# A fused spectral mixer and feed-forward kernel: three edits of the order of work (turning of a tile, mixing tables and first rows, third weight chunk)

## The chip, the core and the metric

The kernel runs on one core of one Trainium2 chip. The metric is the device time of the core in microseconds (us), as the median of several runs. The engines are TensorE (PE in the rows, PEld its weight loads), VectorE (DVE), ScalarE (ACT), GpSimd (POOL) and SyncE (SP), which here only issues DMAs. Each engine works through its own list in order, and they meet at semaphores.

## The reference

Two stages, both in float32:

```python
X = rfft(x, axis=1)                     # x: 4 x 3008 x 256
Yr = Xr @ w_r - Xi @ w_i + b_r          # complex mixing over the 256 features
Yi = Xr @ w_i + Xi @ w_r + b_i
Y  = soft_threshold(Yr, 0.01) + 1j * soft_threshold(Yi, 0.01)
y  = irfft(Y, n=3008, axis=1)           # 12032 rows of 256
h  = y @ w_in                           # 256 -> 2048
g  = max(h, 0) + alpha * min(h, 0)
out = g @ w_out                         # 2048 -> 256
```

## The kernel before, in words

Every product is made of three matmuls in a rounded format: a value is split into an upper part (`_hi`, mostly a ScalarE copy) and the rest (`_lo`, a subtraction on VectorE or GpSimd), and hi*hi, hi*lo and lo*hi are summed in PSUM.

The feed-forward stage is a loop over 24 tiles `f` (6 for each of the 4 batches, 502 or 500 rows of y each) and, in a tile, over 16 steps `m` of 128 hidden units. On TensorE a step is `hidden(f, m)` (6 matmuls into one of two banks `h_ps`) and, two steps behind (`LAG = 2`), `output` (3 matmuls into each of the two halves of `out_ps`). Between them lie, for step m: ScalarE's `bend` (`rows<-h_ps`, the negative part), VectorE's `bend` (`g_raw`), ScalarE's `split_bent` (`g_hi`), VectorE's `rest_bent` (`g_lo`). When the 16 steps are summed, VectorE turns the two halves of `out_ps` (`turn(f-1, 0)` and `turn(f-1, 1)`, `turned<-out_ps`) at step 1 of the next tile, and `output(f, 0)` may overwrite the first half after turn 0 and the second after turn 1.

The Fourier transforms of the next batch are woven into these steps. The order is written out by hand in each engine's loop, with functions that say what lies at which step: `s_unit` (first forward stage: `x_hi`, `x_lo`, `forward1`, `copy_fwd` into `staging`), `p_unit` and `p_couple` (second stage, mixing), `i_unit` (inverse: `inverse1`, `split_y`, `rest_y`), `i_bpair` (pairs of rows to be loaded by `load_back` and split). The split of a pair of rows is `split_back` on ScalarE (lines 850, 851), `rest_back` on GpSimd (line 1288, of `inv_sb`) and `rest_first` on VectorE (line 1129, of the 32 first rows). Batch 0's transform is done ahead of the loop, in the head.

`ffw` is the pair of weights `w_in`, `w_out`, cut in 8 chunks of 2 steps. SyncE loads a chunk into one of two places in `turned` (`load_ffw`, lines 431 and 433); ScalarE makes `win_hi` and `wout_hi`, VectorE `win_lo` (`rest_win`), GpSimd `wout_lo` (`rest_wout`). In tile 0, chunk `m // 2 + 2` is split at each even step m. `load_ffw(w)` waits until chunks 0 to w - 2 have their rests. The sums and differences of the mixing weights for the later batches are made on GpSimd at tile 1, step 0, and split by `split_mixw` (ScalarE) and `rest_mixw` (GpSimd). Rests on VectorE have line 991, those on GpSimd line 1239.

Of the kernel before, what the change touches and what calls it, by code (L numbers as in the profile page):

```python
# [62 lines left out]
LAG = 2  # L63
PERIOD = 6 * STEPS
CHUNKS = 8

ALONE = (1, TILES * STEPS - 1)


# [36 lines left out]

def i_split(f, m):

    return i_bpair(f, 0) if m == 2 else i_bpair(f, m - 1) if m > 2 else None


def i_bpair(f, m):

    pairs = next_bpairs(f)
    return pairs[m // 4] if m % 4 == 0 and m // 4 < len(pairs) else None


def mixer_kernel(nc, x, w_r, w_i, b_r, b_i, w_in, w_out, alpha, dft, idft, twiddles, out):
    with ExitStack() as ctx:
# [227 lines left out]
        def _(sp):  # L347
# [125 lines left out]

            for f in range(TILES):
                for m in range(STEPS):
                    if f == 0 and m % 2 == 0 and m >= 2:
                        load_ffw(m // 2 + 3)
                    if f == 0 and m == STEPS - 1:
                        sp.wait_ge(win_lo_done, CHUNKS)
                        sp.wait_ge(wout_lo_done, CHUNKS)  # L480
                        sp.wait_ge(itw_lo_done, GROUPS)
                        for c in range(2):
                            sp.dma_start(ffw_raw(1)[:, c * 2 * DIM:(c + 1) * 2 * DIM].rearrange("p (h e) -> p h e", h=DH),
                                         (w_r, w_i)[c].rearrange("(h p) e -> p h e", h=DH)).then_inc(mixw_again, 16)
                            sp.dma_start(bias_both[:, c, :], (b_r, b_i)[c].rearrange("(o e) -> o e", o=1).to_broadcast([P, DIM])
                                         ).then_inc(both_loaded, 16)
                    if f >= 1 and 4 <= m < 10:
                        store_out(sp, f - 1, 2 * (m - 4))
                        store_out(sp, f - 1, 2 * (m - 4) + 1)
                    s = s_unit(f, m)  # L490
                    if s is not None:
                        store_fwd(sp, s)
                        load_x(s + X_RING)
                    if f % 6 == 1 and m == 2 and f < TILES - 6:
                        for j in range(4):
                            load_pair(PAIRS * (f // 6 + 1) + j)
                    p = p_unit(f, m, 0)
                    if p is not None:
                        if p % PAIRS + 4 < PAIRS:
                            load_pair(p + 4)  # L500
                    p = p_unit(f, m, 2)
                    if p is not None and p % 3 == 0:
                        load_table(p // 3 + 1)
                    p = p_couple(f, m, 6)
                    if p is not None:
                        store_couple(p)
                    v = i_bpair(f, m)
                    if v is not None:
                        load_back(v)
# [235 lines left out]
        def _(act):  # L745
# [185 lines left out]
                split_back(v)  # L931
            for u in HEAD_ORDER:
                split_y(u)
            act.wait_ge(win_hi_done, 2)
            act.wait_ge(wout_hi_done, 2)
            for f in range(TILES):
                for m in range(STEPS):
                    q = f * STEPS + m
# [8 lines left out]
                    s = s_unit(f, m)  # L947
                    if s is not None:
                        copy_fwd(s)
                    if f == 1 and m in (1, 2):  # L950
                        split_mixw(m)
                    p = p_couple(f, m, 5)
                    if p is not None:
                        copy_couple(p)
# [12 lines left out]
                    v = i_split(f, m)  # L967
                    if v is not None:
                        split_back(v)
                    if f == 0 and m % 2 == 0 and m // 2 + 2 < CHUNKS:  # L970
                        split_ffw(m // 2 + 2)
                    p = p_unit(f, m, 0)
                    if p is not None:
                        split_whole(p)
# [14 lines left out]
        def _(dve):  # L989
# [191 lines left out]
                    split_x(S_HEAD + (k - 19) // 2, True)  # L1181
            for s in range(S_HEAD + 2, S_EARLY):
                split_x(s, True)
            for v in range(HEAD_V):
                rest_back(v)
            for u in HEAD_ORDER:
# [5 lines left out]
            for f in range(TILES):  # L1192
                for m in range(STEPS):
                    if f >= 1 and m == LAG - 1:
                        turn(f - 1, 0)
                    q = f * STEPS + m
                    if q in ALONE:
                        rest_bent(*divmod(q - 1, STEPS))
                    bend(f, m)
                    p = p_unit(f, m, 0)  # L1200
                    if p is not None:
                        whole_spec(p)
                    if q >= 1 and q not in ALONE:
                        rest_bent(*divmod(q - 1, STEPS))
                    if f >= 1 and m == LAG - 1:
                        turn(f - 1, 1)
# [14 lines left out]
                    p = p_unit(f, m, 0)  # L1221
                    if p is not None:
                        rest_whole(p)
                    if f == 0 and m % 2 == 0 and m // 2 + 2 < CHUNKS:
                        rest_win(m // 2 + 2)
                    p = p_couple(f, m, 3)
                    if p is not None:
                        rest_couple(p)
                    v = i_bpair(f, m - 2)
                    if v is not None:  # L1230
                        rest_first(v)
            rest_bent(TILES - 1, STEPS - 1)
# [4 lines left out]
        def _(pool):  # L1237
# [70 lines left out]
            for p in (PAIRS - 2, PAIRS - 1):  # L1308
                for b in (4, 5):
                    hand_over(pool, p, b, head_handed)  # L1310
            pool.wait_ge(wout_lo_done, 2)
            for f in range(TILES):
                for m in range(STEPS):
                    p = p_unit(f, m, 0)
# [2 lines left out]
                    if f == 1 and m == 0:  # L1317
                        make_mixw(1)
                        make_mixw(2)
                    if f == 1 and m in (1, 2):  # L1320
                        rest_mixw(m)
                    p = p_unit(f, m, -2)
                    if p is not None and p % 3 == 0:
                        rest_tw(p // 3)
# [6 lines left out]
                    p = p_unit(f, m, 0)  # L1331
                    if p is not None:
                        rest_sum(p)
                    if f == 0 and m % 2 == 0 and m // 2 + 2 < CHUNKS:
                        rest_wout(m // 2 + 2)
                    if s_unit(f, m + 2) is not None:
                        rest_x(s_unit(f, m + 2))
            for n in (9, 10, 11):
# [68 lines left out]
```

## Time and profile before

| | us |
|---|---|
| median of 3 runs | 1391.45 (1390.62 to 1391.94) |
| the profiled execution | 1391.81 |
| its span, first to last instruction | 1389.8 |
| TensorE busy in it | 1365.3 |
| VectorE, ScalarE, GpSimd busy | 1028.2, 763.1, 318.5 |
| mean granted TensorE clock | 0.994 |

The profiled execution is one run; its own time is 0.36 us over the median, and 2.0 us of it lie outside the span. Durations in this text come from that execution.

### The profile page before, as it was taken

The page shows a single profiled execution, that of the slowest core. Times are in us where ns is not written, and L with a number is a line of the kernel's source. Part 1 is how long each engine was busy: PE and PEld are TensorE (multiplying, and loading weights), DVE is VectorE, ACT ScalarE, POOL GpSimd, SP SyncE. Part 2 cuts the span into 40 slices and gives each one's busy share as a digit, 9 for nine tenths or more (in the row PEclk, how much of TensorE's full clock was granted, in tenths as well). Part 3 has the DMA queues.
Part 4 walks back from the last instruction along what each step waited for, and adds up shares of the span by engine and source line. Part 5 has one row for each costly group of instructions (what it writes and reads, how often), then busy time and mean ns, then how long its engine had stood idle before and what let it go on. Part 6 is the DMA issues. An engine that isn't in the chain of part 4 may idle for free.

```text
span 1389.8 us, 21671 instructions
## 1 busy us (share of the span) xinstructions
PE 1365.3 (98%) x6906; PEld 1156.2 (83%) x6906; DVE 1028.2 (74%) x1887; ACT 763.1 (55%) x1709; POOL 318.5 (23%) x361
## 2 busy tenths in 40 slices
PE   7999999999999999999999999999999999999997
PEld 4987888888888888888888888888888888888886
DVE  6776788888866768989876667888886566566654
ACT  4775566665644555666644545666564444444443
POOL 1443432332200422333210332323220000000000
PEclk9999999999999999999999999999999999999999
DMA  8654532232211542323211343232311121102101
GB/s 257 180 152 138 156 86 72 74 80 84 53 44 31 145 126 60 81 71 83 59 49 42 82 116 86 66 79 77 87 43 41 28 49 39 24 26 49 27 16 15
DMA packets 174700, 106.85 MB, mean 77 GB/s; under 512 B 112198, under 2 KB 150390, under 8 KB 174587
## 3 DMA queue, kind: packets, MB, share of 16 engines
q1 hardware_dynamic: 170755, 101.64, 27.4%
q10 hardware_dynamic: 3608, 3.66, 0.8%
q8 instruction: 56, 0.92, 0.3%
q14 instruction: 57, 0.47, 0.1%
q0 software_dynamic: 224, 0.16, 0.1%
HBM read 67.87 MB, written 37.49 MB: 76 GB/s over the span
## 4 chain that ended last, share of the span: by engine, by line
PE 92%; DVE 4%; issue 1%; ACT 1%; DMA 1%; POOL 0%; SPq 0%; POOLq 0%; DVEq 0%; ACTq 0%
PE out_ps L525 39%; PE h_ps L525 37%; PE work_ps L525 11%; PE work_ps L631 2%; PE work_ps L559 1%; PE work_ps L633 1%; DVE x_lo L991 1%; DVE g_lo L991 1%; PE work_ps L560 1%; DVE g_raw L1092 1%; DVE turned L1146 0%; DVE x_hi L999 0%; PE h_ps L690 0%; DMA room<-in_twiddles_dram 0%; DVE shr_lo L991 0%
## 5 line engine op out<-in xcount | busy, mean ns | idle before, releaser
L865 ACT ACTIVATE rows<-h_ps 128x502 f32<-128x502 f32 (+1 forms) x384 | 225.8, 588 | 522.0 <-PE h_ps L525 522.0
L1092 DVE SCALAR_TENSOR_TENSOR g_raw<-rows,keep,h_ps 128x502 f32<-128x502 f32 (+1 forms) x384 | 280.9, 732 | 271.5 <-ACT rows L865 267.6
L525 PE MATMUL out_ps<-g_hi,wout_hi 128*128 128x502 f32 (+1 forms) x768 | 307.3, 400 | 3.0 <-DVE g_lo L991 2.0
L525 PE MATMUL h_ps<-y_hi,win_hi 128*128 128x502 f32 (+1 forms) x768 | 300.7, 392 | 0.1
L525 PE MATMUL h_ps<-y_lo,win_hi 128*128 128x502 f32 (+1 forms) x768 | 300.3, 391 | 0.0
L525 PE MATMUL out_ps<-g_hi,wout_lo 128*128 128x502 f32 (+1 forms) x768 | 299.8, 390 | 0.0
L525 PE MATMUL h_ps<-y_hi,win_lo 128*128 128x502 f32 (+1 forms) x768 | 299.3, 390 | 0.0
L525 PE MATMUL out_ps<-g_lo,wout_hi 128*128 128x502 f32 (+1 forms) x768 | 299.0, 389 | 0.0
L991 DVE TENSOR_TENSOR g_lo<-g_raw,g_hi 128x502 fp32r<-128x502 f32 (+1 forms) x384 | 273.6, 713 | 1.0 <-ACT g_hi L874 0.7
L874 ACT ACTIVATE g_hi<-g_raw 128x502 fp32r<-128x502 f32 (+1 forms) x384 | 236.9, 617 | 1.7 <-DVE g_raw L1092 1.7
L525 PEld LDWEIGHTS out_ps<-g_hi,wout_hi 128*128 128x128 f32 x768 | 144.9, 189 | 33.6 <-DVE g_lo L991 10.0
L525 PEld LDWEIGHTS h_ps<-y_hi,win_hi 128*128 128x128 f32 x768 | 145.5, 189 | 30.9 <-issue 0.5
L525 PEld LDWEIGHTS h_ps<-y_hi,win_lo 128*128 128x128 f32 x768 | 144.8, 189 | 30.9
L525 PEld LDWEIGHTS out_ps<-g_hi,wout_lo 128*128 128x128 f32 x768 | 144.8, 189 | 30.1
L525 PEld LDWEIGHTS h_ps<-y_lo,win_hi 128*128 128x128 f32 x768 | 145.1, 189 | 29.7
L525 PEld LDWEIGHTS out_ps<-g_lo,wout_hi 128*128 128x128 f32 x768 | 145.6, 190 | 21.1
L1239 POOL TENSOR_TENSOR back_lo<-inv_sb,back_lo 128x256 fp32r<-128x256 f32 x61 | 54.5, 893 | 414.3 <-ACT back_lo L851 414.3
L1261 POOL TENSOR_TENSOR room<-room 128x128 f32<-128x128 f32 x72 | 60.1, 835 | 324.8 <-DVE room L1015 324.8
L1239 POOL TENSOR_TENSOR x_lo<-x_raw,x_hi 94x512 fp32r<-94x512 f32 x44 | 59.2, 1346 | 89.6 <-DVE x_hi L999 89.6
L525 PE MATMUL work_ps<-mixw_hi,spec_hi 128*128 128x256 f32 x216 | 61.5, 285 | 0.0
L525 PE MATMUL work_ps<-mixw_lo,spec_hi 128*128 128x256 f32 x216 | 61.0, 282 | 0.0
L525 PE MATMUL work_ps<-mixw_hi,spec_lo 128*128 128x256 f32 x216 | 60.9, 282 | 0.0
(143 smaller groups left out, 2007.8 us busy)
## 6 DMA issues: line engine op xcount, KB each, us to landing
pair_raw<-fwd_scratch SPq DMA_DIRECT2D x96, 128.0 KB, 2.2
rows<-inv_scratch SPq DMA_DIRECT2D x61, 192.0 KB, 2.4
table<-in_twiddles_dram SPq DMA_DIRECT2D x28, 384.0 KB, 3.4
inv_scratch<-inv_sb SPq DMA_DIRECT2D x36, 256.0 KB, 2.2
x_raw<-in_x_dram SPq DMA_DIRECT2D x56, 160.0 KB
fwd_scratch<-staging SPq DMA_DIRECT2D x46, 192.0 KB, 2.1
inv_sb<-inv_scratch SPq DMA_DIRECT2D x122, 64.0 KB, 2.3
out_dram<-turned SPq DMA_DIRECT2D x124, 40.0 KB, 1.8
```

Of the source, the lines that this page charges most:

```text
L525: mm = pe.matmul(ps, lhs, rhs, start=(first and n == 0), stop=(last and n == len(terms) - 1), **kw)
L559: pe.matmul(both, hi, tw.rearrange("p w c -> p (w c)"), start=True, stop=False, skip_group_check=True)
L560: mm = pe.matmul(both[:, 0:P], lo, tw[:, 0, :], start=False, stop=True, skip_group_check=True)
L631: pe.matmul(i_bank(u)[:, b * 2 * NA:(b + 1) * 2 * NA], back_hi[:, v % 2, d], parts, start=b == 0, stop=False, skip_group_check=True)
L633: pe.matmul(i_views(u)[0], back_lo[:, v % 2, h * P:(h + 1) * P], idft_rest[:, :, :], start=False, stop=True, skip_group_check=True).then_i ...
L865: act.activation(negpart[:, q % 2, 0:size], h_ps[:, q % 2, 0:size], ACT.Relu, scale=-1.0).then_inc(negpart_done, 1)
L874: act.activation(g_hi[:, q % 3, 0:size], g_raw[:, q % 2, 0:size], ACT.Copy).then_inc(g_hi_done, 1)
L991: return dve.tensor_tensor(dst, whole, hi.bitcast(F32), ALU.subtract)
L1092: dve.scalar_tensor_tensor(g_raw[:, q % 2, 0:size], negpart[:, q % 2, 0:size], keep[:, m:m + 1], h_ps[:, q % 2, 0:size], ALU.mult, ALU.add ...
L1239: return pool.tensor_tensor(dst, whole, hi.bitcast(F32), ALU.subtract)
L1261: pool.tensor_tensor(spec_sum, spec[:, :, 0, :], spec[:, :, 1, :], ALU.add).then_inc(sum_done, 1)
```

## The change

Four things are moved; no arithmetic is added or dropped.

1. At step 1 of each tile from 1 on (`m == LAG - 1`), VectorE makes `g_lo` of the step before ahead of `g_raw` of this one.
2. The mixing tables are split at steps 3 and 4 of tile 1, not 1 and 2. The first pair of rows of tile 0 is split at step 3, not 2.
3. The third weight chunk (number 2) is split by VectorE alone in the head, ahead of `rest_back`, and not at step 0 of tile 0.
4. In tile 0, step m issues the load of chunk m/2 + 4 from step 0 on, where before it was chunk m/2 + 3 from step 2 on.

```diff
+FFW_HEAD = 3
 def i_split(f, m):
-    return i_bpair(f, 0) if m == 2 else i_bpair(f, m - 1) if m > 2 else None
+    first = 3 if f == 0 else 2
+    return i_bpair(f, 0) if m == first else i_bpair(f, m - 1) if m > first else None
+def i_first(f, m):
+    return i_bpair(f, 0) if m == (3 if f == 0 else 2) else i_bpair(f, m - 2) if m > 2 else None
+def ffw_unit(f, m):
+    w = m // 2 + 2
+    return w if f == 0 and m % 2 == 0 and FFW_HEAD <= w < CHUNKS else None
...
 # sync
-                    if f == 0 and m % 2 == 0 and m >= 2:
-                        load_ffw(m // 2 + 3)
+                    if f == 0 and m % 2 == 0:
+                        load_ffw(m // 2 + 4)
...
 # scalar
-            act.wait_ge(win_hi_done, 2)
-            act.wait_ge(wout_hi_done, 2)
+            act.wait_ge(win_hi_done, FFW_HEAD)
+            act.wait_ge(wout_hi_done, FFW_HEAD)
...
-                    if f == 1 and m in (1, 2):
-                        split_mixw(m)
+                    if f == 1 and m in (3, 4):
+                        split_mixw(m - 2)
...
-                    if f == 0 and m % 2 == 0 and m // 2 + 2 < CHUNKS:
-                        split_ffw(m // 2 + 2)
+                    w = ffw_unit(f, m)
+                    if w is not None:
+                        split_ffw(w)
...
 # vector
+            for step in range(4):
+                split_ffw(2, step)
             for v in range(HEAD_V):
                 rest_back(v)
...
-                    if q in ALONE:
+                    g_first = q in ALONE or m == LAG - 1
+                    if g_first:
                         rest_bent(*divmod(q - 1, STEPS))
                     bend(f, m)
...
-                    if q >= 1 and q not in ALONE:
+                    if q >= 1 and not g_first:
                         rest_bent(*divmod(q - 1, STEPS))
...
-                    v = i_bpair(f, m - 2)
+                    v = i_first(f, m)
                     if v is not None:
                         rest_first(v)
```

GpSimd's `rest_wout` and `rest_mixw` and VectorE's `rest_win` follow in the same way.

Three places show how the lists of the engines differ; the changed kernel's lines lie 14 to 19 further down. The first is SyncE's queue in tile 0, steps 0 to 4, in the kernel before. A line with `turned` is half of a weight chunk's load, the group of `rows` and `inv_sb` is one `load_back`.

```order
L406 DMA rows<-inv_scratch 96x512 [waits inv_stored_1,inv_stored_2,inv_stored_0,back_lo_done]
L408 DMA rows<-inv_scratch 32x512
L411 DMA inv_sb<-inv_scratch 64x256 x2
L431 DMA turned<-in_moe_w_in_dram 128x2x256 [waits wout_lo_done,win_lo_done]
L433 DMA turned<-in_moe_w_out_dram 128x2x256
L431 DMA turned<-in_moe_w_in_dram 128x2x256 [waits wout_lo_done,win_lo_done]
L433 DMA turned<-in_moe_w_out_dram 128x2x256
L406 DMA rows<-inv_scratch 96x512 [waits back_part_done,back_lo_done]
L408 DMA rows<-inv_scratch 32x512
L411 DMA inv_sb<-inv_scratch 64x256 x2
```

The same stretch in the changed kernel:

```order
L445 DMA turned<-in_moe_w_in_dram 128x2x256 [waits wout_lo_done,win_lo_done]
L447 DMA turned<-in_moe_w_out_dram 128x2x256
L420 DMA rows<-inv_scratch 96x512 [waits inv_stored_1,inv_stored_2,inv_stored_0,back_lo_done]
L422 DMA rows<-inv_scratch 32x512
L425 DMA inv_sb<-inv_scratch 64x256 x2
L445 DMA turned<-in_moe_w_in_dram 128x2x256 [waits wout_lo_done,win_lo_done]
L447 DMA turned<-in_moe_w_out_dram 128x2x256
L445 DMA turned<-in_moe_w_in_dram 128x2x256 [waits wout_lo_done,win_lo_done]
L447 DMA turned<-in_moe_w_out_dram 128x2x256
L420 DMA rows<-inv_scratch 96x512 [waits back_part_done,back_lo_done]
L422 DMA rows<-inv_scratch 32x512
L425 DMA inv_sb<-inv_scratch 64x256 x2
```

The load of chunk 4 now stands ahead of the first `load_back`, and two chunk loads, 5 and 6, not 4 and 5, stand ahead of the second. The guard of each names the same semaphores with the count one chunk higher for a step.

The second place is VectorE at step 1 of tile 1, where tile 0 is turned; here before, from turn 0 to `g_raw` of step 2.

```order
L1146 STREAM_TRANSPOSE turned<-out_ps 128x5x3x32 [waits wout_lo_done,out_half]
L1146 STREAM_TRANSPOSE turned<-out_ps 128x32
L1092 SCALAR_TENSOR_TENSOR g_raw<-rows,keep,h_ps 128x502 [waits g_lo_done,g_hi_done,negpart_done]
L991 TENSOR_TENSOR g_lo<-g_raw,g_hi 128x502 [waits g_hi_done]
L1146 STREAM_TRANSPOSE turned<-out_ps 128x5x3x32 [waits out_mm]
L1146 STREAM_TRANSPOSE turned<-out_ps 128x32
L1092 SCALAR_TENSOR_TENSOR g_raw<-rows,keep,h_ps 128x502 [waits g_lo_done,g_hi_done,negpart_done]
```

And in the changed kernel:

```order
L1161 STREAM_TRANSPOSE turned<-out_ps 128x5x3x32 [waits wout_lo_done,out_half]
L1161 STREAM_TRANSPOSE turned<-out_ps 128x32
L1006 TENSOR_TENSOR g_lo<-g_raw,g_hi 128x502 [waits g_hi_done]
L1107 SCALAR_TENSOR_TENSOR g_raw<-rows,keep,h_ps 128x502 [waits g_lo_done,g_hi_done,negpart_done]
L1161 STREAM_TRANSPOSE turned<-out_ps 128x5x3x32 [waits out_mm]
L1161 STREAM_TRANSPOSE turned<-out_ps 128x32
L1107 SCALAR_TENSOR_TENSOR g_raw<-rows,keep,h_ps 128x502 [waits g_lo_done,g_hi_done,negpart_done]
```

`g_lo` and the first `g_raw` have changed places between the two turns.

The third place is GpSimd's list from the first step of tile 0 to step 5, before:

```order
L1239 TENSOR_TENSOR wout_lo<-turned,wout_hi 128x512 [waits wout_hi_done,wout_lo_done]
L1239 TENSOR_TENSOR back_lo<-inv_sb,back_lo 128x256 [waits back_hi_done]
L1239 TENSOR_TENSOR wout_lo<-turned,wout_hi 128x512 [waits wout_hi_done]
L1239 TENSOR_TENSOR x_lo<-x_raw,x_hi 94x512 [waits x_hi_done]
L1239 TENSOR_TENSOR wout_lo<-turned,wout_hi 128x512 [waits wout_hi_done]
L1239 TENSOR_TENSOR x_lo<-x_raw,x_hi 94x512 [waits x_hi_done]
L1239 TENSOR_TENSOR back_lo<-inv_sb,back_lo 128x256 [waits back_hi_done]
L1239 TENSOR_TENSOR x_lo<-x_raw,x_hi 94x512 [waits x_hi_done]
```

And in the changed kernel, in which the rest of chunk 2 (the first line above) is no longer there, so that the list begins with chunk 3:

```order
L1258 TENSOR_TENSOR wout_lo<-turned,wout_hi 128x512 [waits wout_hi_done,wout_lo_done]
L1258 TENSOR_TENSOR back_lo<-inv_sb,back_lo 128x256 [waits back_hi_done]
L1258 TENSOR_TENSOR x_lo<-x_raw,x_hi 94x512 [waits x_hi_done]
L1258 TENSOR_TENSOR wout_lo<-turned,wout_hi 128x512 [waits wout_hi_done]
L1258 TENSOR_TENSOR x_lo<-x_raw,x_hi 94x512 [waits x_hi_done]
L1258 TENSOR_TENSOR back_lo<-inv_sb,back_lo 128x256 [waits back_hi_done]
L1258 TENSOR_TENSOR x_lo<-x_raw,x_hi 94x512 [waits x_hi_done]
```

The rest of the first rows (`back_lo`) has moved behind the rest of chunk 3; at step 5 `back_lo` stands ahead of `x_lo` as before.

## Rows read from the trace of the kernel before

**Rows 1.** The page, busy time of the tensor engine (us, share, instructions).
```profile
PE 1365.3 (98%) x6906; PEld 1156.2 (83%) x6906; DVE 1028.2 (74%) x1887; ACT 763.1 (55%) x1709; POOL 318.5 (23%) x361
```

**Rows 2.** Waits: who waited for whom; us, times, longest us.
```profile
PEld out_ps L525 <- DVE g_lo L991: 10.0, 20, 1.3
PEld out_ps L525 <- DVE turned L1146: 2.8, 15, 0.2
```

**Rows 3.** Timeline, tile 22, steps 1 to 3: start us, us, engine, operation [idle, releaser].
```profile
1294.86 0.78 DVE L1146 STREAM_TRANSPOSE turned<-out_ps 128x480 f32<-128x480 f32 x2 [1.47 <-PE out_ps L525]
1295.56 0.70 DVE L1092 SCALAR_TENSOR_TENSOR g_raw<-rows,keep,h_ps 128x502 f32<-128x502 f32 x1
1296.18 0.67 DVE L991 TENSOR_TENSOR g_lo<-g_raw,g_hi 128x502 fp32r<-128x502 f32 x1
1296.77 0.77 DVE L1146 STREAM_TRANSPOSE turned<-out_ps 128x480 f32<-128x480 f32 x2
...
1296.91 0.50 PE L525 MATMUL out_ps<-g_hi,wout_hi 128*128 128x502 f32 x1
...
1298.38 0.39 PE L525 MATMUL h_ps<-y_hi,win_hi 128*128 128x502 f32 x1
```

**Rows 4.** Timeline, tile 1, steps 1 to 3, GpSimd, vector and tensor engine.
```profile
175.79 1.28 POOL L1239 TENSOR_TENSOR mixw_lo<-biased,mixw_hi 128x512 fp32r<-128x512 f32 x1 [0.79 <-ACT mixw_hi L804]
...
176.09 1.52 DVE L991 TENSOR_TENSOR g_lo<-g_raw,g_hi 128x502 fp32r<-128x502 f32 x1
177.53 0.77 DVE L1146 STREAM_TRANSPOSE turned<-out_ps 128x480 f32<-128x480 f32 x2
...
179.14 0.39 PE L525 MATMUL h_ps<-y_hi,win_hi 128*128 128x502 f32 x1
```

**Rows 5.** Timeline of the vector engine between the head and its last rests.
```profile
107.56 1.29 DVE L991 TENSOR_TENSOR back_lo<-rows,back_hi 96x512 fp32r<-96x512 f32 x2 [4.93 <-ACT back_hi L847]
```

**Rows 6.** Timeline, tile 0, steps 0 to 2.
```profile
119.27 1.40 POOL L1239 TENSOR_TENSOR wout_lo<-turned,wout_hi 128x512 fp32r<-128x512 f32 x1 [16.15 <-ACT wout_hi L880]
...
119.67 1.55 DVE L991 TENSOR_TENSOR g_lo<-g_raw,g_hi 128x502 fp32r<-128x502 f32 x1
...
121.27 0.50 PE L525 MATMUL out_ps<-g_hi,wout_hi 128*128 128x502 f32 x1 [0.60 <-DVE g_lo L991]
```

**Rows 7.** Timeline, tile 0, steps 2 to 4.
```profile
124.74 1.68 DVE L991 TENSOR_TENSOR back_hi<-rows,back_hi 32x512 fp32r<-32x512 f32 x1
...
127.83 0.50 PE L525 MATMUL out_ps<-g_hi,wout_hi 128*128 128x502 f32 x1 [0.52 <-DVE g_lo L991]
...
129.31 0.39 PE L525 MATMUL h_ps<-y_hi,win_hi 128*128 128x502 f32 x1
```

**Rows 8.** Sync engine's queue, tile 0, step 4; last, line 411: issue to landing.
```profile
125.94 0.37 SPq L431 DMA_DIRECT2D turned<-in_moe_w_in_dram  x1
...
127.84 2.09 SPq L411 DMA_DIRECT2D inv_sb<-inv_scratch  x2
...
DMA to landing us min/median/max: 2.6/3.0/3.4
```

**Rows 9.** Timeline, tile 0, steps 4 to 7.
```profile
132.03 1.36 DVE L991 TENSOR_TENSOR win_lo<-turned,win_hi 128x512 fp32r<-128x512 f32 x1
...
132.35 0.62 ACT L850 ACTIVATE back_hi<-rows 128x512 fp32r<-128x512 f32 x1
...
133.36 0.74 POOL L1239 TENSOR_TENSOR back_lo<-inv_sb,back_lo 128x256 fp32r<-128x256 f32 x1 [0.53 <-ACT back_lo L851]
135.05 1.30 POOL L1239 TENSOR_TENSOR x_lo<-x_raw,x_hi 94x512 fp32r<-94x512 f32 x1 [0.95 <-DVE x_hi L999]
...
137.89 0.39 PE L525 MATMUL work_ps<-x_hi,dft_hi 128*128 128x512 f32 x1
```

**Rows 10.** Windows: us, busy us by engine (count), granted clock, DMA share, GB/s.
```profile
106.00:110.00 4.00, 2.61 (x19) 2.10 (x18) 2.24 (x4) 2.11 (x5) 0.00 (x0) 1.00 0.83 258
111.00:117.50 6.50, 6.50 (x24) 5.85 (x24) 1.50 (x5) 1.12 (x5) 0.00 (x0) 0.50 0.23 74
```

More of the change, by code:

```diff
@@ L1223, in _ @@
                         rest_whole(p)
-                    if f == 0 and m % 2 == 0 and m // 2 + 2 < CHUNKS:
-                        rest_win(m // 2 + 2)
+                    w = ffw_unit(f, m)
+                    if w is not None:
+                        rest_win(w)
                     p = p_couple(f, m, 3)
@@ L1310, in _ @@
                     hand_over(pool, p, b, head_handed)
-            pool.wait_ge(wout_lo_done, 2)
+            pool.wait_ge(wout_lo_done, FFW_HEAD)
             for f in range(TILES):
@@ L1319, in _ @@
                         make_mixw(2)
-                    if f == 1 and m in (1, 2):
-                        rest_mixw(m)
+                    if f == 1 and m in (3, 4):
+                        rest_mixw(m - 2)
                     p = p_unit(f, m, -2)
@@ L1333, in _ @@
                         rest_sum(p)
-                    if f == 0 and m % 2 == 0 and m // 2 + 2 < CHUNKS:
-                        rest_wout(m // 2 + 2)
+                    w = ffw_unit(f, m)
+                    if w is not None:
+                        rest_wout(w)
                     if s_unit(f, m + 2) is not None:
```

## The prediction

> **What bounds the kernel now.** I read the page first: the tensor engine is busy 1365.3 of 1389.8 us [rows 1], so apart from some 24 us only its own work counts, and the change takes no matmul away. It can move the time only through the engine's waits. The list of waits came next. Between the matmuls of the steps the two that the turning of a tile makes are small: 10.0 us on g_lo in 20 places, of which one is 1.3 long, and 2.8 us on the turned blocks in 15 places [rows 2]. So all that the reordering could ever give is a few us, and the question is what each edit does to one wait. For that I read the timeline of a late turn without other traffic [rows 3], the turn of tile 1 [rows 4], and tile 0's first eight steps [rows 5 to 9].
>
> Cadence: in [rows 3] six matmuls take 1298.38 - 1296.91 = 1.47, of which 0.11 is the restart after a wait (0.50 against 0.39), so 0.227 each and 1.36 for a hidden step.
>
> **The turn (22 places, tile 1 aside).** Before, the vector engine does turn 0, g_raw, g_lo, turn 1, back to back from 1294.86 to 1296.77 + 0.77 = 1297.54 [rows 3]. Now it does turn 0, g_lo, g_raw, turn 1: the same four, ending at the same moment. The tensor engine's second half of the output step needs turn 1. Before, the next hidden step starts at 1298.38, 0.84 behind the end of turn 1. The other path ends at the same place: g_lo ends at 1296.85, 1.53 ahead, which is 0.06 of signal, 0.11 of restart and six matmuls. Two paths tie; the change shortens one. I take the gain as 0. Bounds: none below, since ScalarE's g_hi is done before turn 0 ends; above, if turn 1 did not hold, the wait before 1296.91, some 0.3 with its restart (1296.91 less the start 0.227 behind the previous matmul, the same in every odd tile), 15 times: 4.5. g_raw comes 0.6 later, and nobody is short of it: the hidden step that needs its bank starts 1.5 us on.
>
> **Tile 1.** Here the same chain is cut open: g_lo starts at 176.09, 0.30 into GpSimd's rest of the mixing table (175.79 + 1.28), and takes 1.52 in place of 0.67, so turn 1 ends at 177.53 + 0.77 = 178.30 and the next hidden step starts 0.84 on, at 179.14 [rows 4]. With the table in steps 3 and 4 the chain lasts 2.68 as in [rows 3], from 174.77, to 177.45, and the hidden step comes at 178.29: gain 0.85. The two ScalarE splits and two GpSimd rests are moved and not dropped; in steps 3 and 4 no turn stands behind them, and they are needed only by the mixing at step 9. I take 0; the worst is that one g_lo is caught again, the same 0.85. The SBUF page of the Trainium skill ("SBUF — State Buffer", section on the two separate sides) says that the pair of ports is an exclusive lock: whichever of a vector operation with two SBUF inputs and a GpSimd operation starts first holds it to its end. The trace agrees: in [rows 6] g_lo ends 0.55 behind GpSimd's end.
>
> **Third chunk in the head.** Two copies and two rests of 128x512 go where the vector engine is idle for 4.93 us before 107.56 [rows 5]. A rest of nearly that size takes 0.67 [rows 3], so four take 2.7: cost 0, and 2.7 if that cover were gone. In tile 0 this takes GpSimd's 1.40 away from step 0 [rows 6]. g_lo starts at 119.67 and ends at 121.22 = 119.27 + 1.40 + 0.55; alone it ends at 120.34, and the output step, now at 121.27 with 0.60 idle ahead of it, starts on time, 0.76 earlier, without its restart: gain 0.87.
>
> **First rows at step 3.** Before, the vector engine's rest of the first rows sits at 124.74 for 1.68, behind GpSimd, ahead of g_raw and g_lo of step 3, and the output step starts at 127.83, 0.70 late and 0.11 for the restart [rows 7]. That wait goes. But the inverse step at step 4 needs these rows and is now reached at 126.0. ScalarE takes up step 3 at about 123.4, when the hidden step ends (122.75 - 0.87 + 1.36 + 0.2); with bend and g_hi at some 0.5 each and the two copies' 0.92 it ends at about 125.4; then the two rests share the port: 0.69 and 0.74 one behind the other, with x_hi of 0.4 ahead, to 126.9. The inverse waits about 1.1. Net of both: the hidden step of step 5, before at 129.31, comes at 128.7, so the gain up to here is 0.6 and not 0.87 + 0.81. Bounds: 0 and 1.7.
>
> **The loads (the term that decides).** Each weight load is issued one even step earlier: chunk m/2 + 4 at step m. It still waits for the chunk two before it, and that one is now split in the same step. At step 4 the sync engine stands at the load of chunk 6 until chunk 4 has its rests, and the load of rows for pair 4 stands behind it in the queue; before, its guard was chunk 3, split two steps earlier, and this queue never waited. The rests of chunk 4 ended at 132.03 + 1.36 = 133.39 [rows 9]. Now: rest of the first rows to 126.9; g_raw 0.7; g_lo, held behind x_lo, to 128.6; x_hi and the two y pieces to 129.6; then win_lo, held by wout_lo's 1.3 from 129.0, ends 0.55 behind it: 130.8. With the contention as before it is 132.8 (the old end less 0.6). The six DMAs from there: 125.94 to the second inv_sb load at 129.3, which lands 2.6 later, 131.9: 6.0 us [rows 8]. So ScalarE, which had its rows in time at 132.35 [rows 9], stands from 131.9 to 136.9 in step 5, with bend and g_hi of steps 6 and 5, copy_fwd and y_hi behind it. GpSimd is in order too: back_lo, then x_lo: 1.01 + 0.74 + 1.30 + 0.15 behind 136.9 [rows 9], that is 140.1. The forward step at step 7, before at 137.89, is reached at 137.25: it waits **2.85**. Behind it the vector engine is late with one x_lo and one g_lo: I put 0.9 on two further waits at step 8 (bounds 0 and 1.5). If the issue is as quick as for the rows alone, 1.0 for the pair in place of 2.09, the wait is 1.8; with the rests at 132.8 it is 4.8.
>
> **Sum.** -0.6 + 2.85 + 0.9 - 0.85 + 0 = +2.3. The profiled execution took 1391.81 (span 1389.8 and 2.0 around it), so 1394.1; it lies 0.36 over the median of 1391.45, so the forecast for the median is **1393.8**. From the bounds (wait 1.8 to 4.8, first steps 0 to 1.7, follow-up 0 to 1.5) its own range is 1392.3 to 1396.0.
>
> **Rivals.**
> (1) The clock falls as well. [Rows 10]: after 106 to 110, with 2.61 of 4.00 us busy in short matmuls, the granted clock is 0.50 (the 1.2 GHz level) from 111 to 117.5. A wait of 2.85 leaves a stretch as empty. For each 3 us at that level half is lost, 1.5, part of it covering the follow-ups: 1395.0. Against it: the stretch around the wait is otherwise full. The page "TensorE: Matmul & The Clock Gate" of the Trainium skill, section "Why this matters for your kernels", asks for no idle gaps over about 3 us; by that 2.85 just passes and the sum stays 1393.8, where the row, with its longest gap near 1.4, leaves a fall open.
> (2) The wait in the queue is absorbed: the rests of chunk 4 come by 127.5 or the rows are not needed until step 8. Then only -0.6 - 0.85 is left: 1390.0. For it: the inverse that uses these rows stands in step 8. Against it: ScalarE and GpSimd have other work queued behind them. This is the rival on the other side; it decides if less than 1.4 us of wait is left at step 7.
> (3) Each turn gains 0.3, as turn 1 does not hold: 15 times 0.3 = 4.5 less than the forecast: 1389.3. Against it: the tie in [rows 3].
> (4) Nothing moves, the terms cancel: 1391.5.
>
> **How the numbers follow.** Forecast 0.50; clock falls 0.25; absorbed 0.15; turns gain 0.03; cancelled 0.07. 0.2% is 2.8 us, about what a measurement of this kernel can tell from no change, so slower starts at 1394.2 and faster at 1388.7. Of the forecast's 0.50 some 0.20 lies over 1394.2, of the clock's 0.25 some 0.19: slower 0.39. Faster has only a little of absorbed and turns: 0.03. Same: 0.58. The range 1390.5 to 1396.0 leaves out about half of absorbed, the turns, and the top of the clock's: 2 in 10.
>
> **What would show it.** At step 4 of tile 0 the sync engine's weight load issued at about 130.9, the row loads behind it; ScalarE idle some 5 us before back_hi, released by the DMA of inv_sb; the tensor engine idle 2 to 3 us ahead of a forward matmul near 137 to 140, released by GpSimd's x_lo. The g_lo of step 0 at 0.67; the output step of tile 0, step 2 on time. At the odd turns the wait moved from g_lo to turned, with the next hidden step at the same distance. In tile 1 the turn without its 1.52. The forecast is wrong if the row load is issued before 128, if the wait at step 7 is under 1.4 or over 4.8, or if the clock row shows 0.50 after 120.

## The result and the profile after

The changed kernel takes **1394.19 us** (median of 13 runs, 1390.88 to 1396.46), the kernel before, beside it, 1391.62 (13 runs, 1390.39 to 1392.56). The ratio is 1.0018, 95% interval 1.0011 to 1.0025: slower by 2.6 us. The interval leaves out 1, so the loss is real, though it lies under the 0.2% that the prediction took as its own threshold. Forecast were 1393.8 and a loss of 2.35. The profiled execution of after took 1396.1 (span 1394.0), 1.9 over its median; that of before (1391.81) lay 0.19 over the median beside it. So 4.2 of difference in span between the two profiles stand for 2.6 between the medians, and what is compared below is places, not totals.

The page of after, tensor engine's busy time, answers to [rows 1]; the waits of its weight loads answer to [rows 2] (us, times, longest us):

```profile
PE 1366.6 (98%) x6906; PEld 1157.0 (83%) x6906; DVE 1025.6 (74%) x1890; ACT 762.4 (55%) x1707; POOL 319.2 (23%) x360
```

```profile
PEld out_ps L539 <- DVE turned L1161: 7.6, 15, 0.6
...
PEld work_ps L539 <- POOL x_lo L1258: 3.5, 5, 2.0
...
PEld out_ps L539 <- DVE g_lo L1006: 2.1, 3, 0.8
```

The wait on `g_lo` went from 10.0 to 2.1 and that on `turned` from 2.8 to 7.6, again 15 times: the waits at the turns changed names. New is 2.0 us in one place on GpSimd's `x_lo`.

The timeline of tile 22, steps 1 to 3, beside [rows 3] (start us, us, engine, operation, [idle, releaser]):

```profile
1298.86 0.78 DVE L1161 STREAM_TRANSPOSE turned<-out_ps 128x480 f32<-128x480 f32 x2 [1.47 <-PE out_ps L539]
...
1299.57 0.64 DVE L1006 TENSOR_TENSOR g_lo<-g_raw,g_hi 128x502 fp32r<-128x502 f32 x1
...
1300.13 0.73 DVE L1107 SCALAR_TENSOR_TENSOR g_raw<-rows,keep,h_ps 128x502 f32<-128x502 f32 x1
...
1300.77 0.77 DVE L1161 STREAM_TRANSPOSE turned<-out_ps 128x480 f32<-128x480 f32 x2
...
1301.60 0.50 PE L539 MATMUL out_ps<-g_hi,wout_hi 128*128 128x502 f32 x1
...
1302.39 0.39 PE L539 MATMUL h_ps<-y_hi,win_hi 128*128 128x502 f32 x1
```

Turn 1 ends at 1301.54; the restart (0.50 for 0.39) now stands half an output step later, ahead of the second half; the hidden step comes 0.85 behind the end of turn 1, before 0.84. Nothing is gained. Tile 1, beside [rows 4]:

```profile
180.16 0.64 DVE L1006 TENSOR_TENSOR g_lo<-g_raw,g_hi 128x502 fp32r<-128x502 f32 x1
...
181.36 0.77 DVE L1161 STREAM_TRANSPOSE turned<-out_ps 128x480 f32<-128x480 f32 x2
...
182.98 0.40 PE L539 MATMUL h_ps<-y_hi,win_hi 128*128 128x502 f32 x1
```

`g_lo` takes 0.64 in place of 1.52. Turn 1 ends at 182.13, and the hidden step comes 0.85 behind it, as in tile 22.

Tile 0, steps 0 to 8 of after, every engine, beside [rows 6 to 9]:

```profile
119.70 0.68 DVE L1006 TENSOR_TENSOR g_lo<-g_raw,g_hi 128x502 fp32r<-128x502 f32 x1 [0.69 <-ACT g_hi L888]
...
127.92 0.44 PE L645 MATMUL work_ps<-idft_parts,back_hi 128*128 128x188 f32 x2 [0.82 <-POOL back_lo L1258]
...
130.41 1.39 DVE L1006 TENSOR_TENSOR win_lo<-turned,win_hi 128x512 fp32r<-128x512 f32 x1
...
131.82 0.37 SPq L445 DMA_DIRECT2D turned<-in_moe_w_in_dram  x1
...
132.80 0.41 SPq L420 DMA_DIRECT2D rows<-inv_scratch  x1
...
133.72 1.09 SPq L425 DMA_DIRECT2D inv_sb<-inv_scratch  x2
...
137.05 0.63 ACT L864 ACTIVATE back_hi<-rows 128x512 fp32r<-128x512 f32 x1 [4.18 <-DMA inv_sb<-inv_scratch]
...
138.06 0.73 POOL L1258 TENSOR_TENSOR back_lo<-inv_sb,back_lo 128x256 fp32r<-128x256 f32 x1 [5.12 <-ACT back_lo L865]
...
138.76 1.27 POOL L1258 TENSOR_TENSOR x_lo<-x_raw,x_hi 94x512 fp32r<-94x512 f32 x1
...
139.15 1.42 DVE L1006 TENSOR_TENSOR g_lo<-g_raw,g_hi 128x502 fp32r<-128x502 f32 x1
...
140.08 0.51 PE L539 MATMUL work_ps<-x_hi,dft_hi 128*128 128x512 f32 x1 [1.61 <-POOL x_lo L1258]
...
145.74 0.49 PE L539 MATMUL out_ps<-g_hi,wout_hi 128*128 128x502 f32 x1 [0.64 <-DVE g_lo L1006]
152.41 0.51 PE L539 MATMUL work_ps<-x_hi,dft_hi 128*128 128x512 f32 x1 [0.23 <-POOL x_lo L1258]
161.61 0.49 PE L539 MATMUL out_ps<-g_hi,wout_hi 128*128 128x502 f32 x1 [0.64 <-DVE g_lo L1006]
```

Read it as one chain: `win_lo` of chunk 4 ends at 131.80; the load of chunk 6, which waited for it, is issued at 131.82; the rows of pair 4 stand behind it in SyncE's queue, at 132.80, though nothing else held them; they land at 137.0; ScalarE has stood 4.18 us; GpSimd's `back_lo` and then its `x_lo` follow; the forward matmul of step 7 starts at 140.08. The three waits after it are smaller. Taking the start of each hidden step of tile 0 and subtracting that of before gives 0.09 at step 0, 0.41 at step 7, 2.28 at step 8, 3.46 at step 9, 3.96 at step 11, 4.68 at step 13 and at the end of the tile. Tile 1 gives 0.85 back, and the rest of the kernel, up to the end of the span, changes it by 0.3.

The granted clock, in windows of after and, in the second fence, of before, beside [rows 10] (us, busy us of PE, PEld, DVE, ACT, POOL with counts, granted clock, DMA share, GB/s):

```profile
106.00:110.00 4.00, 2.84 (x21) 2.34 (x19) 2.32 (x5) 2.33 (x5) 0.00 (x0) 1.00 0.88 270
111.00:117.50 6.50, 6.50 (x24) 5.85 (x25) 1.44 (x5) 0.98 (x3) 0.00 (x0) 0.50 0.52 146
117.50:121.00 3.50, 3.50 (x11) 2.78 (x11) 1.79 (x3) 1.80 (x3) 0.00 (x0) 0.58 0.00 0
```

```profile
117.50:121.00 3.50, 3.09 (x12) 1.91 (x11) 2.67 (x3) 2.91 (x6) 1.40 (x1) 0.96 0.01 2
```

The stretch at the 1.2 GHz level lasted 6.8 us in this profile of before (111.0 to 117.8) and 10.2 in after's (110.2 to 120.4). After 121 the clock did not fall again in after until the last 4 us of the span, also not behind the wait at step 7.

### The profile page after: what moved, and what is told of

The parts are those of the page before. It is cut to its first block, busy times and chain, and to the rows that moved or that the text cites. A ratio compares the mean times of both kernels' runs of the same rounds, so it can differ in the third digit from the quotient of the medians.

```text
span 1394.0 us, 21671 instructions
## 1 busy us (share of the span) xinstructions
PE 1366.6 (98%) x6906; PEld 1157.0 (83%) x6906; DVE 1025.6 (74%) x1890; ACT 762.4 (55%) x1707; POOL 319.2 (23%) x360
## 4 chain that ended last, share of the span: by engine, by line
PE 90%; DVE 4%; issue 2%; DMA 1%; ACT 1%; SPq 0%; POOL 0%; DVEq 0%; POOLq 0%; ACTq 0%
PE out_ps L539 38%; PE h_ps L539 37%; PE work_ps L539 11%; PE work_ps L645 2%; PE work_ps L573 1%; DVE turned L1161 1%; PE work_ps L647 1%; DVE g_lo L1006 1%; PE work_ps L574 1%; DVE x_lo L1006 1%; DVE x_hi L1014 0%; PE h_ps L704 0%; DMA room<-in_twiddles_dram 0%; DMA fwd_scratch<-staging 0%; DVE shr_lo L1006 0%
## 5 line engine op out<-in xcount | busy, mean ns | idle before, releaser
L1006 DVE TENSOR_TENSOR g_lo<-g_raw,g_hi 128x502 fp32r<-128x502 f32 (+1 forms) x384 | 268.5, 699 | 1.5 <-ACT g_hi L888 1.4
```

The costliest lines, as they stand in the source:

```text
L1006: return dve.tensor_tensor(dst, whole, hi.bitcast(F32), ALU.subtract)
```

## The experiments

Two theories were held against each other for the loss. **Queue**: the rows of pair 4 stand behind the guarded weight load in SyncE's queue, and ScalarE and GpSimd behind the rows. **Traffic**: three chunks of weights are on the way early, and DMAs, vector engine and GpSimd get in each other's way, whatever the order in the queue. A third question was what the head's stretch at half clock does to every run. Ratios are to the kernel before, run in the same session, and can be set side by side; medians of two experiments can come from different sessions.

**1. The changed kernel with the old load schedule.**

```diff
-                    if f == 0 and m % 2 == 0:
-                        load_ffw(m // 2 + 4)
+                    if f == 0 and m % 2 == 0 and m >= 2:
+                        load_ffw(m // 2 + 3)
```

> The changed kernel with the weight loads of tile 0 issued as before (chunk m/2 + 3 from step 2 on), all else kept. Queue theory (the loss is the row load standing behind a chunk load whose guard is not yet met): the waits at steps 7, 8, 10 and the longer one at 12 go, ScalarE no longer idles 4 us before back_hi at step 5; what is left are the gains, 0.6 in tile 0's first steps and 0.85 in tile 1, so 1.0 to 1.7 us under the kernel before, about 1390.1. Clock theory (the loss is a longer spell at 1.2 GHz around 110 to 120 us, whatever the loads): the time stays near 1394, and its runs spread over some 5 us as those of the changed kernel.

Measured 1390.21 (12 runs, 1385.65 to 1391.97), ratio 0.9991 (0.9978 to 1.0003): 4.0 below after, whose interval lies wholly above. Among runs whose mean granted clock was 0.995 the means are 1391.8 for before (13 runs), 1390.5 here (6), and 1394.9 for after (7, in its own session). Part 4 of the change makes the whole loss and more. The other parts together come to -1.3 at equal clock, where the forecast had -0.6 - 0.85; the interval of the ratio contains 1, so this gain over before is not clear of noise.

**2. The chunk in the head and the early loads alone** (before, with parts 3 and 4 of the change).

> The kernel before with two of the edits: third chunk in the head, and chunk loads one even step earlier. Turn, mixing tables and first rows as before. Queue theory: the head gives 0.9 at step 2, the first rows at step 2 keep their wait at step 4, and the row load for pair 4 is held as in the changed kernel: a wait of 2 to 3 us before a forward matmul at step 7 and about 1 behind it. No gain in tile 1. 2.5 to 4 us over the kernel before, about 1394.8. Clock theory: as the kernel before or anywhere up to 1396, with the excess in the slow spell before 121 us and not at step 7.

Measured 1397.12 (5 runs, 1394.96 to 1397.66), ratio 1.0046 (1.0031 to 1.0061). The forward matmul of step 7 and the clock behind it:

```profile
140.74 0.50 PE L539 MATMUL work_ps<-x_hi,dft_hi 128*128 128x512 f32 x1 [3.87 <-POOL x_lo L1258]
```

```profile
141.00:145.00 4.00, 4.00 (x12) 3.17 (x12) 3.90 (x6) 1.84 (x4) 2.97 (x2) 0.57 0.13 34
```

The queue's chain ends 0.66 later than in after, but the tensor engine comes there 1.6 earlier, so it waits 3.87, and then the clock goes to half for 3.4 us from 141.3 (the window has the mean 0.57). This is rival 1 of the prediction, seen in a kernel with a longer wait than after's: hidden step 7 still starts 1.2 ahead of before, hidden step 8 4.2 behind, 5.4 in one step, of which 4.0 are the wait with its restart and the other 1.4 the clock. The expectation had 2.5 to 4 us over before and no fall of the clock: the loss came out as 5.8, with only 5 runs.

**3. Turns alone** (part 1) and **4. mixing tables alone** (the first half of part 2).

```diff
-                    if q in ALONE:
+                    g_first = q in ALONE or m == LAG - 1
+                    if g_first:
...
-                    if q >= 1 and q not in ALONE:
+                    if q >= 1 and not g_first:
```

> The kernel before with the turn's reordering alone (g_lo ahead of g_raw at step 1 of tiles 1 to 23). Tie theory: the waits move from g_lo to the turned blocks and the hidden step of step 3 starts as early as before in all tiles but tile 1, where g_lo gets the port ahead of GpSimd's rest of the mixing table: 0.85 less, about 1390.7. Rival (each turn gains 0.3): 4.5 less, about 1387. Rival (the later g_raw holds up ScalarE and the next step): 1 us or more over.

Measured 1390.67 (12 runs), ratio 1.0000 (0.9991 to 1.0010).

```diff
-                    if f == 1 and m in (1, 2):
-                        split_mixw(m)
+                    if f == 1 and m in (3, 4):
+                        split_mixw(m - 2)
...
-                    if f == 1 and m in (1, 2):
-                        rest_mixw(m)
+                    if f == 1 and m in (3, 4):
+                        rest_mixw(m - 2)
```

> The kernel before with the mixing tables split at steps 3 and 4 of tile 1 alone. g_lo at the turn of tile 0 takes 0.67, not 1.52; the hidden step of step 3 of tile 1 starts 0.85 earlier and nothing is lost at steps 3 to 5: about 1390.4. As the reordered turn alone gives the same 0.85 there, the two together give it once. Rival (the table's rests catch another g_lo): as before, 1391.3.

Measured 1390.74 (12 runs), ratio 0.9997 (0.9988 to 1.0007). Both profiles gain the same in tile 1, steps 1 to 2, 0.85 and 0.83, and nothing in the 22 other turns. Either of the two edits is enough: one takes `g_lo` out of GpSimd's way, the other GpSimd out of `g_lo`'s. The total is too small for the timing: neither ratio is clear of 1. Among runs at clock 0.995 the means differ from before's by -0.7 and -1.0.

**5. The kernel before once more**, as its own control.

> The kernel before, unchanged, for the clock of each of its runs and a second profile. Expected ratio 1.000. If the slow spells in the head are a matter of chance alone, its runs show mean clocks that differ as much as those of the changed kernel (0.994 to 0.998) and a spread of 5 us; the 13 runs so far spread over 2.2 us only. If the spread belongs to the change, the clocks stay within 0.001 and the times within 2.5 us.

Measured 1391.07 (12 runs, 1388.57 to 1393.43), ratio 1.0003 (0.9993 to 1.0013). Its profile has the stretch at half clock 10.2 long, not 6.8, and two waits on `g_lo` at steps 8 and 12 that the first profile of the same kernel has not: it ends 1.6 later.

```profile
143.19 0.49 PE L525 MATMUL out_ps<-g_hi,wout_hi 128*128 128x502 f32 x1 [0.39 <-DVE g_lo L991]
...
158.83 0.49 PE L525 MATMUL out_ps<-g_hi,wout_hi 128*128 128x502 f32 x1 [0.77 <-DVE g_lo L991]
```

So single profiles of this kernel differ by that much. The 12 runs spread over 4.9 us, at mean clocks from 0.994 to 0.999: the wide spread belongs to the kernel before as well and not to the change.

**6. The changed kernel with the weight load behind the rows in the queue.** All loads stay early; the two lines of part 4 only move behind the step's `load_back`.

> The changed kernel with its early chunk loads, but in each even step of tile 0 the chunk load stands behind the row load in the sync engine's list. Queue theory (head of line): the row load for pair 4 goes out near 127 again, ScalarE's 4.2 us ahead of back_hi at step 5 and the waits at steps 7 and 8 are gone; as with the loads undone, about 1390.2, 3.5 to 4.5 under the changed kernel. Rival (the early loads themselves hurt, by their traffic or by keeping a place in turned): it stays over 1393.

Measured 1389.96 (12 runs, 1386.12 to 1391.72), ratio 0.9988 (0.9979 to 0.9997). SyncE's queue and ScalarE at steps 3 to 5:

```profile
123.96 0.33 SPq L420 DMA_DIRECT2D rows<-inv_scratch  x1
...
127.89 0.40 SPq L445 DMA_DIRECT2D turned<-in_moe_w_in_dram  x1
...
128.83 0.62 ACT L864 ACTIVATE back_hi<-rows 128x512 fp32r<-128x512 f32 x1
```

The rows go out 4 us ahead of the weight load, ScalarE has no wait for them, and the loss is gone though the weights come as early. This decides between the theories: the order in the queue, not the traffic. (This profile had no stretch at half clock around 110 us, which puts it ahead of the others from the start; the missing wait is read within it, and the ratio is over all runs.)

**7. The changed kernel with pairs 4 and 5 split a step later** on ScalarE and GpSimd; queue and loads as in after.

```diff
-    return i_bpair(f, 0) if m == first else i_bpair(f, m - 1) if m > first else None
+    later = 2 if f == 0 else 1
+    return i_bpair(f, 0) if m == first else i_bpair(f, m - later) if m > first else None
```

> The changed kernel with the splits of pairs 4 and 5 of tile 0 one step later (ScalarE and GpSimd at steps 6 and 10 in place of 5 and 9); the row load is as late as in the changed kernel. Queue theory in its second half (the loss is what stands behind the split on ScalarE and GpSimd, not the rows themselves, which are used at step 8): x_lo of step 5 is done near 133, no wait at step 7, at most 1 us at steps 7 to 9; 1390.2 to 1391.5. Rival (the rows themselves are late for the tensor engine): 1393 to 1395, with the wait moved to the inverse at step 8.

Measured 1392.17 (12 runs), ratio 1.0006 (0.9998 to 1.0015): 2.0 below after.

```profile
136.45 0.63 ACT L865 ACTIVATE back_hi<-rows 128x512 fp32r<-128x512 f32 x1 [0.49 <-DMA inv_sb<-inv_scratch]
...
141.67 0.50 PE L540 MATMUL work_ps<-x_hi,dft_hi 128*128 128x512 f32 x1 [0.32 <-POOL x_lo L1259]
...
149.73 0.50 PE L540 MATMUL work_ps<-x_hi,dft_hi 128*128 128x512 f32 x1 [0.58 <-POOL x_lo L1259]
```

The rows are as late as in after, but ScalarE waits 0.49 for them, not 4.18, and the wait of step 7 is gone; two small ones stand at steps 8 and 10. About half of the loss was thus made in the second queue (by the ratios 0.12% of 0.27%): other work stood behind the split of late rows on ScalarE and GpSimd. More was left than expected (1390.2 to 1391.5): the waits at steps 8 and 10 cost 0.6 and 0.9 with their restarts.

**8. The third chunk in the head alone** (part 3) and **9. the first rows alone** (the second half of part 2).

> The kernel before with the third chunk's split in the head alone; chunk loads, first rows, turn and tables as before. The output step of tile 0, step 2, starts on time: 0.87 gained there and kept, as the profile with the loads moved as well showed from step 2 to 3; the wait at step 4 stays at 0.8 to 0.9. About 1390.4. Against the kernel with both, 1397.1, it tells what the early loads cost: 6 to 7 us.

Measured 1391.62 (12 runs), ratio 1.0004 (0.9996 to 1.0013); at clock 0.995 1392.1 against 1392.0. The forecast gain of 0.87 does not show. The wait of step 3 is what is left in its profile:

```profile
127.84 0.49 PE L539 MATMUL out_ps<-g_hi,wout_hi 128*128 128x502 f32 x1 [0.72 <-DVE g_lo L1006]
```

It was 0.52 in [rows 7]; the stretch at half clock is 10.2 long here, and its hidden steps start 0.66 behind before at step 2 and 0.23 ahead at step 3. With the clock low so long, the wait of [rows 6] isn't there in the kernel before either: in experiment 5 the same two numbers are 0.91 and 0.28. So 0.6 of the 0.87 is only to be had in runs with a short stretch. Set against experiment 2, which is this kernel with the early loads added, the early loads cost 5.5 here, not 4.0.

> The kernel before with the first pair of rows of tile 0 split at step 3 alone. The wait of 0.7 and its restart before the output at step 4 goes, a wait before the inverse at step 4 takes its place, of up to 1 us, since the rows come later; net 0.3 faster to 0.3 slower at step 5, so 1391.3 within 0.3. Rival (the move is a gain by itself): 0.8 less, 1390.5.

Measured 1391.37 (12 runs), ratio 1.0003 (0.9994 to 1.0012).

```profile
125.79 0.44 PE L637 MATMUL work_ps<-idft_parts,back_hi 128*128 128x188 f32 x2 [0.82 <-POOL back_lo L1245]
```

The wait of step 3 is gone, and this one at step 4 has come in its place, 0.3 longer in the balance (hidden step 5 against hidden step 3). Alone this edit is a swap.

**10. The old load schedule, and the tensor engine kept busy in the head.** The kernel has `stay_warm(n)`, n matmuls whose result nobody reads, to fill gaps. Here there are more of them around 106 to 111 us (the diff leaves out the loads, which are those of experiment 1).

```diff
-            stay_warm(12)
+            stay_warm(18)
...
-                if u in (2, 1):
-                    stay_warm(1)
+                if u in (0, 2, 1, 3):
+                    stay_warm(2)
```

> The changed kernel with the loads of before, and in the head 6 more idle matmuls ahead of the first inverses (18 in place of 12) and two after each of four of the inverses in place of one after two. Clock theory (the spell at 1.2 GHz from 110 us on follows the stretch of 106 to 110 us in which the tensor engine idles and runs short matmuls, and costs half of 7 to 10 us): no spell there, mean clock 0.997 or more in nearly all runs, 1386 to 1388, against 1390.2. Rival (the added matmuls hold up the inverses, or the spell comes anyway): 1390 to 1392.

Measured 1388.37 (11 runs, 1387.18 to 1389.09), ratio 0.9981 (0.9972 to 0.9990).

```profile
106.00:110.00 4.00, 3.97 (x24) 3.25 (x23) 2.25 (x4) 2.26 (x5) 0.00 (x0) 1.00 0.87 269
111.00:117.50 6.50, 6.14 (x34) 4.80 (x34) 2.23 (x6) 2.15 (x6) 0.00 (x0) 1.00 0.38 123
```

With 3.97 of 4.00 busy the clock stays at 1.00, and the spread of the runs goes from 6.3 us (experiment 1) to 1.9; every run has a mean granted clock of 0.997 or more. The median came 0.4 above the range expected, for the fillers have a price of their own. In experiment 6's profile, which had no stretch near 110 us either and has no added fillers, tile 0 begins 1.13 earlier; first its first hidden step, then that of this run:

```profile
112.48 0.46 PE L539 MATMUL h_ps<-y_hi,win_hi 128*128 128x502 f32 x1
```

```profile
113.61 0.46 PE L539 MATMUL h_ps<-y_hi,win_hi 128*128 128x502 f32 x1
```

The 1.1 stays to the end (spans 1385.0 and 1386.2). The fastest run here is 1387.18, where experiment 1 had one of 1385.65: the fillers take away the slow runs and also the fastest ones. The interval overlaps with that of experiment 1, so the gain over it, 1.8 in the medians of two sessions, is likely but not shown.

**11. Old load schedule, and the vector engine's rests of the first rows of tile 0 at steps 3, 7 and 11.**

```diff
-    return i_bpair(f, 0) if m == (3 if f == 0 else 2) else i_bpair(f, m - 2) if m > 2 else None
+    if f == 0:
+        return i_bpair(f, m - 3) if m > 2 else None
+    return i_bpair(f, m - 2) if m >= 2 else None
```

> The changed kernel with the loads of before and VectorE's rests of the first rows in tile 0 at steps 3, 7 and 11 in place of 3, 6 and 10. The wait at step 12 (0.2 to 0.8 before an output, on g_lo queued behind that rest) goes, and none takes its place as the inverse that needs the rows stands one step on: 0.2 to 0.8 less than 1390.2. Rival: the inverse at step 8 or 12 waits for the rest, no gain.

Measured 1389.11 (12 runs, 1386.10 to 1390.51), ratio 0.9987 (0.9978 to 0.9997). The rest takes 0.69 at each later place, where it took 1.67 beside GpSimd, and the wait of step 12 is gone. That wait was short (0.29 before a weight load in experiment 1's profile); that the median lies 1.1 under experiment 1, in another session, is more than it explains, and the intervals overlap.

**12. Experiments 10 and 11 together.**

> The kernel with the fillers of the head (the run with stay_warm(18) and stay_warm(2) behind the inverse passes, loads of the weight chunks as before), and in tile 0 the rests of the first rows at steps 3, 7 and 11 as in the run that moved them. Theory (what is left in the head after the clock is held is the wait for g_lo at step 12, 0.18 us in that run's profile): median 1388.2, at most 0.3 below the 1388.37 of the run with fillers alone, granted clock 0.997 or more in every run, and no stretch at 0.50 before the last 10 us. Rival (the 1.1 us between the moved rests and the old table was mostly the chance of the clock, and a rest at step 3 delays the row cast): the same as the run with fillers within 0.2, or 0.3 above it. Both have it below both kernels by over 0.2%.

Measured 1389.02 (11 runs, 1388.34 to 1390.65), ratio 0.9986 (0.9977 to 0.9995), clock 0.997 or more in every run. It is below both kernels, but not below experiment 10: the two gains do not add up, and the median is even 0.65 above it, more than theory or rival had, which the intervals, overlapping, do not tell from nothing. The lowest median and ratio are those of experiment 10, though the intervals do not set it apart from experiments 1, 6, 11 and 12; by the two ratios, 0.9981 and 1.0018, it lies 0.37% or 5.1 us under after.

## Why the prediction held, point by point

**Turns: 0.** Shown. In after and in experiment 3 the waits moved from `g_lo` to `turned` at the same distance; rival 3 is out.

**Tile 1: -0.85.** Shown, 0.85 in after, and from either edit alone.

**Start of tile 0: -0.6.** Right only for executions like the one it was read from. From hidden step 0 to hidden step 5 the profiles of experiments 7 and 11, with a stretch of 6.8 like that of [rows 10], gain 0.59 and 0.60 on before. That of experiment 1, with a stretch of 10.2, gains 0.2; after's own, also with 10.2, loses 0.3. The step that failed there is "the output step starts on time, 0.76 earlier": the wait of 0.60 in [rows 6] isn't there in the kernel before either when the stretch is long (experiment 5). The other two halves were right: `g_lo` alone took 0.68, and the wait on the inverse at step 4 was 0.98 with its restart, where 1.1 was forecast; experiments 8 and 9 give nothing measurable each in the medians. The cover in the head, 4.93 idle in [rows 5], was there.

**The queue: 2.85 at step 7, chain end 140.1.** The chain ended at 140.08, but two of its links were off and cancelled: the rests of chunk 4 came at 131.80, not 130.8, as `win_lo` met GpSimd's rest and ran 1.39 from 130.41; and the `inv_sb` pair issued in 1.09, not 2.09. The wait cost 1.87 with its restart, not 2.85, since the tensor engine reached the place 1.05 later than forecast (138.3 for 137.25), which is the start's term again. The place itself is right to 0.03: hidden step 8 was forecast 2.25 behind before and came 2.28 behind. Experiments 1 and 6 show that the loss comes from the early loads, and by their place in the queue; experiment 7 shows that ScalarE's and GpSimd's order makes half of it. Rival 2, which took the late rows as harmless because they are used at step 8, was wrong: the work queued behind their split was not free.

**Follow-ups: 0.9, bounds 0 and 1.5.** Mis-sized against the profile it was forecast from: 2.40, of which 1.2 at step 8, 0.5 at step 10, 0.7 at step 12. The prediction counted only step 8 and took the rest of tile 0 as before. But experiment 5 has two such waits, 0.6 and 0.8, in the unchanged kernel, and against that profile after loses only 0.80 here. What these waits are in a typical run stays open. In medians the early loads cost 4.0, at equal clock 4.4; the forecast had 3.75 (2.85 + 0.9). In the kernel before with the head edit alone (experiments 2 and 8) they cost 5.5.

**The clock falls too, rival 1.** Not in after's profile: clock 1.00 from 121 on. (The prediction's sign of being wrong, 0.50 after 120, was met by 0.4 us, but by the tail of the head's stretch and not by a fall behind the wait.) In experiment 2 it fell behind a wait of 3.87. The section "Why this matters for your kernels" of the page "TensorE: Matmul & The Clock Gate" in the Trainium skill wants no idle gap over about 3 us. By that the gap of 3.87 loses the clock and after's of 1.61 does not, and the traces agree in both; they do not agree at 106 to 110, where the longest gap is 1.39 in before and 1.16 in after and the clock falls all the same.

**The total.** The forecast is 0.4 from the median and right in place and sign, but part of that is luck. It was made from the profile of before, and against that profile the after profile is 4.2 longer, not 2.3: 0.4 up to step 7, 1.87, 2.40, -0.85 and 0.3 later on. Against the profile of experiment 5, whose stretch at half clock is as long as after's, the difference is 2.6, as in the medians: -0.2 ahead of tile 0, 0.33 up to step 7, 1.87, 0.80, -0.84, and 0.6 in the later tiles, which is not explained. In this pairing the start is worse than forecast by 0.9 and the wait at step 7 better by 1.0; the two errors cancel. The stated range of the prediction, 1392.3 to 1396.0, is also narrower than its bounds: added up they give 1390.7 to 1396.9.

## What to carry to other kernels

Before a guarded DMA is issued earlier, look at what stands behind it in the same queue: the guard's wait is handed to every transfer behind it, and from there to whatever stands behind those transfers' consumers on their engines. Put the load that can wait behind those that others need at once. And a wait read in one execution is a term only if the executions agree at that place; where the clock varies upstream, count it for part of the runs. When two single profiles are compared, take two whose clock fell at the same places and for as long. Filling a hole to hold the clock has a price too, here about 1.1 us in an execution that would have kept the clock anyway.

## What the runs showed of the hardware

The granted clock's stretch at 0.50 behind 106 to 110 us varies from one execution of a kernel to the next: in the profiles it was 6.8 or 10.2 us long, and in those of experiments 4 and 6 it was missing. Those two, like the profiles of before and of experiments 2 and 7, had 3.4 us at 0.50 earlier in the head, between 33 and 44 us, which the seven others without added fillers had not; so the mean clock of a run doesn't tell which stretch it had. The spread of the runs goes with the mean clock: in the session of experiments 1 to 3 and 5 the runs of the kernel before had a mean of 1391.8 at clock 0.995 (13 runs), 1389.7 at 0.997 (6) and 1388.2 at 0.998 (3). Before this stretch the tensor engine had been busy 2.61 (before) and 2.84 us (after) of 4.00 in short matmuls, and 2.86 and 2.73 in the two executions without the stretch: the same emptiness costs the clock in one execution and not in another. With 3.97 (experiment 10) and 4.00 (experiment 12) it did not come. That the mean clock and not something else beside it sets these times is only read from this order and from experiments 10 and 12.
